# An attention, Fourier-mixing and gated feed-forward kernel: the last 64 tokens of two batches share one output tile, the gated part is unrolled, and the stages stand in a new order

## The reference, cut to what matters

```python
# attention: 4 batches x 8 heads, 576 tokens, head size 64
out_d = softmax(q_d @ k_d.T * scale) @ v_d        # on means over 4 tokens, repeated 4 times
out_l = softmax(q @ k.T * scale, |i - j| < 4) @ v # local band
x = transpose(out_up + out_l)                     # 4 x 576 x 512
# mixing layer
u = x + real(fft(fft(x, axis=1), axis=2))
un = (u - mean(u)) / sqrt(var(u) + 1e-6)
x = u + relu(un @ w_ch1) @ w_ch2                  # 512 -> 2048 -> 512
# gated layer
h = relu(x @ w_in)                                # 512 -> 1024
conv = sum_k conv_w[k] * shift(h, k - 1)          # over tokens, 3 taps, zeros at the ends
out = (h * sigmoid(conv)) @ w_out                 # 1024 -> 512
```

## Time and profile before

| | us |
|---|---|
| median of 3 runs | 891.83 |
| lowest, highest | 890.42, 895.41 |
| profiled execution | 889.25 |
| its span, first to last instruction | 887.4 |

### The profile page before, as it was taken

The page is one execution under the profiler, slowest core; times in us unless marked ns, Lnnn a source line. Parts: engine busy times, 40 slices in busy tenths (PEclk is TensorE's granted clock), DMA queues, the critical chain, the costliest instruction groups (busy, mean ns, idle before and its releaser), DMA issues.

```text
span 887.4 us, 17493 instructions
## 1 busy us (share of the span) xinstructions
PE 855.7 (96%) x6884; PEld 792.4 (89%) x6884; DVE 474.4 (53%) x889; ACT 333.6 (38%) x1040; POOL 266.8 (30%) x272
## 2 busy tenths in 40 slices
...
GB/s 181 271 90 61 69 88 65 38 52 110 70 25 69 40 51 69 119 1 25 24 154 91 30 31 30 30 31 31 31 31 1 1 54 2 2 51 0 53 0 54
DMA packets 75492, 49.41 MB, mean 56 GB/s; under 512 B 59201, under 2 KB 64601, under 8 KB 75418
## 3 DMA queue, kind: packets, MB, share of 16 engines
...
...
## 4 chain that ended last, share of the span: by engine, by line
PE 82%; DVE 7%; ACT 4%; issue 2%; POOL 1%; SPq 1%; DMA 1%; ACTq 0%; DVEq 0%; POOLq 0%
PE banks L744 21%; PE banks L761 21%; PE banks L860 13%; PE banks L845 10%; PE banks L702 3%; PE banks L675 3%; PE banks L592 2%; PE banks L651 2%; PE banks L717 1%; PE banks L573 1%; ACT prob L901 1%; PE banks L614 1%; DMA qk_in<-in_q 1%; ACT cent L963 1%; PE banks L635 1%
## 5 line engine op out<-in xcount | busy, mean ns | idle before, releaser
L1199 DVE SCALAR_TENSOR_TENSOR hL<-banks,hH 128x256 fp32r<-128x256 f32 x144 | 60.3, 419 | 185.6 <-ACT hH L959 185.6
L959 ACT ACTIVATE hH<-banks 128x256 fp32r<-128x256 f32 x144 | 55.1, 383 | 253.3 <-PE banks L744 253.1
L1486 POOL TENSOR_TENSOR astage<-astage,rstd_bc 128x1024 f32<-128x1024 f32 x9 | 21.6, 2399 | 228.8 <-DVE astage L1329 228.8
L744 PE MATMUL banks<-unH,w1aH 128*128 128x256 f32 x288 | 86.9, 302 | 2.2 <-DVE hL L1199 2.1
L761 PE MATMUL banks<-hH,w2aH 128*128 128x256 f32 x288 | 83.6, 290 | 0.0
L744 PE MATMUL banks<-unH,w1bH 128*128 128x256 f32 x288 | 82.5, 287 | 0.0
L744 PE MATMUL banks<-unL,w1bH 128*128 128x256 f32 x288 | 82.1, 285 | 0.0
L761 PE MATMUL banks<-hH,w2bH 128*128 128x256 f32 x288 | 82.0, 285 | 0.0
L761 PE MATMUL banks<-hL,w2bH 128*128 128x256 f32 x288 | 82.0, 285 | 0.0
L761 PE MATMUL banks<-hH,w2bL 128*128 128x256 f32 x288 | 82.0, 285 | 0.0
L744 PE MATMUL banks<-unH,w1bL 128*128 128x256 f32 x288 | 82.0, 285 | 0.0
...
## 6 DMA issues: line engine op xcount, KB each, us to landing
...
acc_dram<-astage SPq DMA_DIRECT2D x9, 512.0 KB, 2.6
astage<-acc_dram SPq DMA_DIRECT2D x9, 512.0 KB, 3.3
out<-ostage SPq DMA_DIRECT2D x4, 1024.0 KB, 4.4
w2araw<-in_moe_w_ch SPq DMA_DIRECT2D x4, 512.0 KB, 8.2
```

Of the source, the lines that this page charges most:

```text
L744: last = nc.tensor.matmul(bank[0][:, 0:CT], w[wp][:, t, P * m:P * m + P], (unH, unL)[xp][:, t, :], start=(t == 0 and i == 0), stop=(t == P ...
L959: nc.scalar.activation(hH[:, m % 2, :], bank[0][:, 0:CT], ACT.Relu).then_inc(hH_ok, 1)
L1199: nc.vector.scalar_tensor_tensor(hL[:, m % 2, :], bank[0][:, 0:CT], 0.0, hH[:, m % 2, :].bitcast(F32), ALU.max, ALU.subtract).then_inc(hL_ ...
L1486: nc.gpsimd.tensor_tensor(astage[:], astage[:], rstd_bc[:].unsqueeze(1).to_broadcast([P, PB, CT]), ALU.mult).then_inc(scaled, 1)
```

## The change

It has three parts.

The unpaired tile of 64 tokens goes. Rounded parts of a batch's last 64 tokens are kept for all 8 slices in `remH` and `remL`, an even batch's in the first 64 columns and the following odd batch's in the other 64. The odd batch contracts these 128 tokens as one tile, before its own four, and two stores take it out. Full tiles and the remainder are rounded by separate instructions.

The gated loop over batches is written out for every engine, and each tile gets its own store, which waits only for its own copy.

`PLAN` is replaced by another order of the same stages, with other counts of fillers (81 calls before, 69 after). Nothing else is added to it or taken from it. The diff of `PLAN` is some 150 lines; here its start stands, and then the places of which the prediction speaks, from the new list.

```diff
-        NTO = (S + P - 1) // P
-        SPAD = NTO * P
+        FULL = S // P
+        REM = S - FULL * P
+        SF = FULL * P
         NG = 4
-        hgH = sb("hgH", [P, NG, SPAD], F32R)
-        hgL = sb("hgL", [P, NG, SPAD], F32R)
-        ostage = sb("ostage", [P, NTO, D])
+        hgH = sb("hgH", [P, NG, SF], F32R)
+        hgL = sb("hgL", [P, NG, SF], F32R)
+        remH = sb("remH", [P, M2, 2 * REM], F32R)
+        remL = sb("remL", [P, M2, 2 * REM], F32R)
+        ostage = sb("ostage", [P, FULL + 1, D])
...
+        def o_tiles(b):
+            return (FULL, 0, 1, 2, 3) if b % 2 else (0, 1, 2, 3)
...
-            with sp.Fori(0, B) as b:
-                sp.wait_ge(o_kept_a, 3 * b + 3)
-                sp.wait_ge(o_kept_v, 2 * b + 2)
-                full = S // P
-                sp.dma_start(out[b][0:full * P].rearrange("(t p) d -> p t d", p=P),
-                             ostage[:, 0:full]).then_inc(o_stored, 16)
-                sp.dma_start(out[b][full * P:S], ostage[0:S - full * P, full]).then_inc(o_stored, 16)
+            for b in range(B):
+                for i, tt in enumerate(o_tiles(b)):
+                    if tt % 2:
+                        sp.wait_ge(o_kept_v, 2 * b + tt // 2 + 1)
+                    else:
+                        sp.wait_ge(o_kept_a, kept_a(b) + (1 if tt == FULL else tt // 2 + 1 + b % 2))
+                    if tt < FULL:
+                        sp.dma_start(out[b][P * tt:P * tt + P], ostage[:, tt]).then_inc(o_stored, 16)
+                    else:
+                        sp.dma_start(out[b - 1][SF:S], ostage[0:REM, tt]).then_inc(o_stored, 16)
+                        sp.dma_start(out[b][SF:S], ostage[REM:P, tt]).then_inc(o_stored, 16)
...
-                for tt in range(NTO):
+                for tt in o_tiles(b):
...
                     for i, (wp, xp) in enumerate(THREE):
-                        last = nc.tensor.matmul(bank[tt][:, :], (hgH, hgL)[xp][:, m % NG, P * tt:P * tt + P],
-                                                (woH, woL)[wp][:, m, :], start=(m == 0 and i == 0),
+                        tokens = ((hgH, hgL)[xp][:, m % NG, P * tt:P * tt + P] if tt < FULL else (remH, remL)[xp][:, m, :])
+                        last = nc.tensor.matmul(bank[tt], tokens, (woH, woL)[wp][:, m, :], start=(m == 0 and i == 0),
                                                 stop=(m == M2 - 1 and i == 2))
...
-                        nc.scalar.copy(hgH[:, n % NG, 0:S], hg[n % 2][:]).then_inc(hgH_ok, 1)
+                        nc.scalar.copy(hgH[:, n % NG, :], hg[n % 2][:, 0:SF])
+                        nc.scalar.copy(remH[:, n, REM * (b % 2):REM * (b % 2) + REM], hg[n % 2][:, SF:S]).then_inc(hgH_ok, 1)
...
-            for slots in (hgH, hgL):
-                nc.vector.memset(slots[:, :, S:SPAD].bitcast(F32), 0.0).then_inc(slots_zero, 1)
...
-                        nc.vector.tensor_tensor(hgL[:, n % NG, 0:S], hg[n % 2][:], hgH[:, n % NG, 0:S].bitcast(F32),
+                        nc.vector.tensor_tensor(hgL[:, n % NG, :], hg[n % 2][:, 0:SF], hgH[:, n % NG, :].bitcast(F32),
+                                                ALU.subtract)
+                        nc.vector.tensor_tensor(remL[:, n, rem], hg[n % 2][:, SF:S], remH[:, n, rem].bitcast(F32),
                                                 ALU.subtract).then_inc(hgL_ok, 1)
```

More of the change, by code:

```diff
@@ L84 @@
[L84 to L113, removed]
@@ L119 @@
[L119 to L133, removed]
@@ new lines @@
+    flip_k.3.0 keep_up.1 flip_k.3.1 keep_k.3.0 round_w1.0.1 weigh.1.0 pool_q.3 load_k.4 keep_k.3.1 pool_k.3 flip_p.2.0
+    pool_v.3 join.1.0 score.3.0 keep_p1.2.0 keep_p0.2.0 score.3.1 mask.3.0 low_w1.0.0 load_vg.4 top_l.3.0 flip_p.2.1
+    mask.3.1 weigh.1.1 exp_l.3.0.0 wmeans.0.1 top_l.3.1 load_vw.3 keep_p1.2.1 low_w1.0.1 top_d.3.0 exp_l.3.0.1
+    keep_p0.2.1 top_d.3.1 exp_d.3.0.0 exp_l.3.1.0 join.1.1 flip_pd.2 fold.1 centre_w1.0.2 exp_l.3.1.1 centre_w1.0.3
+    keep_pd.2 exp_d.3.0.1 flip_q.4.0 flip_q.4.1 exp_d.3.1.0 invert.3.0 pooled.2 load_q.5 exp_d.3.1.1 norm_l.3.0
@@ new lines @@
+    join.3.0 exp_l.4.0.1 flip_k.5.1 keep_k.5.0 load_k.6 weigh.3.1 top_d.4.1 round_w2.0.1 join.3.1 load_vw.5 fold.3
+    pool_q.5 exp_d.4.1.0 exp_d.4.1.1 round_w2.0.2 pool_v.4 fold_d.0.1 invert.4.0 low_w1.0.3 warm.15.1 feat.0.0.0
+    keep_k.5.1 load_vg.5 pool_k.5 feat.0.0.1 keep_cos.0.0 feat.0.1.0 top_l.4.1 keep_sin.0.0 norm_l.4.0 low_w2.0.1
+    exp_l.4.1.0 score.5.0 flip_p.4.0 exp_l.4.1.1 feat.0.1.1 keep_cos.0.1 mask.5.0 keep_p1.4.0 feat.0.2.0 keep_sin.0.1
+    invert.4.1 top_l.5.0 norm_l.4.1 feat.0.2.1 keep_cos.0.2 exp_l.5.0.0 keep_p0.4.0 turn.0.0 seq.0.0.0 top_d.5.0
@@ new lines @@
+    load_k.7 norm_d.5 keep_k.6.0 seq.0.3.1 keep_k.6.1 pool_k.6 mix_p.0.2 flip_p.5.0 keep_qs.0.3 join.4.0 score.6.0
+    keep_p1.5.0 mix.0.3 norm_l.5.1 weigh.4.1 keep_p0.5.0 mask.6.0 mix_p.0.3 load_vw.6 flip_p.5.1 join.4.1 keep_p1.5.1
+    keep_p0.5.1 top_l.6.0 flip_pd.5 fold.4 round_u.0.0 round_u.0.1 low_u.0.0 keep_pd.5 low_u.0.1 top_d.6.0 round_u.0.2
+    flip_q.7.0 round_u.0.3 flip_q.7.1 low_u.0.2 pooled.5 exp_d.6.0.0 low_u.0.3 load_q.8 exp_d.6.0.1 expand.0.0
+    keep_up.5 pool_v.7 exp_l.6.0.0 score.6.1 relu.0.0 exp_l.6.0.1 split.0.0 load_vg.8 weigh.5.0 top_d.6.1 keep_q.7.0
```

285 lines of the change are left out of this document (159 added, 126 removed).

## The result

| | before | after |
|---|---|---|
| median of 20 runs each, same chip (us) | 891.12 | 884.88 |
| lowest to highest | 889.03 to 901.21 | 878.67 to 890.00 |
| profiled execution, its span | 889.25, 887.4 | 886.86, 885.1 |
| mean granted clock in it | 0.982 | 0.967 |

The ratio is 0.9916 (95%: 0.9891 to 0.9941): 7.5 us less by it, 6.2 by the medians, where the prediction gave 18.2 and a range that ended at 881. The gain is in the gated part and at the end. The new order of stages, which was to give 4.9 us, costs some 7.

What follows compares the result with a forecast made beforehand. TensorE, holding 82% of the chain of waits, was taken to bound the kernel. Savings of 11.2 + 2.1 + 4.5 + 0.4 = 18.2 us from the runs' median of 891.83 gave 873.6 us, range 867 to 881.

Steps and rivals of the forecast that it cites:

- The shared tile: Gated part: 432 matmuls instead of 480, 48 fewer at a pitch of 0.2333 us, 11.2 us saved, lower bound 5.8.
- rival 4: Gated part: a matmul that goes frees only a narrow one's pitch, 0.120 us; 879.0 us in all, chance 0.03.
- The split: Gated part: separate instructions add 0.1 us per slice on VectorE or ScalarE, covered by waits; cost 0, at worst 8.
- unrolling: Gated part: writing out the loop wins nothing and costs 0, though more distinct instructions must be fetched.
- Rival 5: Gated part: unrolled code is fed too slowly; 14 ns more per pair cost 17 us, 20 ns give 898; chance 0.03.
- Stores and end: After TensorE's last matmul: a smaller last store lands sooner, 2.1 us saved, bounds 0 and 2.5.
- End of the layer norm: At the layer's end: one centring step stays before the square, which then waits for a relu; 0.4 us saved.
- The front: Before the first transform matmul: the new order closes holes of VectorE; 4.5 us saved, bounds -4 and 7.3.
- sign of being wrong: The first transform matmul starting at 79 us or later, where about 75 was forecast.
- The middle: From 107.8 to 450 us: only 5.6 us of rest can be won; gain 0, bounds -3 and 3.
- to be paid back: Front: three stages slipping behind the transform's start gain some 1.8 us there, an estimate, to be lost again behind it.
- Rival 2: Front or middle loses 4 to 9 us through delayed loads or a lowered clock: 882 to 887, chance 0.08.

Runs made afterwards that it cites:

- e8: The kernel before with the gated part's loops written out for all four batches, nothing else changed: 893.36 us, ratio 1.0010.
- e12: e1 with the stores of the kernel before: 882.3 us, ratio 0.9902.
- e1: The kernel after with the PLAN of the kernel before: 877.0 us, ratio 0.9833.
- e13: The kernel after with the order of before only from the first transform stage to the first expansion: 880.72 us, ratio 0.9875.
- e3: The kernel after with load_vg.2 issued ahead of load_q.3: 884.3 us, ratio 0.9897.

## Why the prediction was wrong

- **The shared tile: right.** 11.2 us forecast, 11.15 in the chain, 432 matmuls. The pitch is 0.233 us, so rival 4 is out. The Trainium skill's figure in "TensorE: Matmul & The Clock Gate", section Back-to-back issue gap, 131 ns, would have made it an estimated 6.3: the trace disagrees.
- **The split, unrolling: right at 0.** The 64-column subtraction took 0.22 us (0.2 assumed). TensorE doesn't rest from its first contraction to its end. Rival 5 is out by e8.
- **Stores and end: right.** 2.1 forecast; the span ends 4.1 us after the last matmul where it was 5.9, so 1.8 less, and 2.3 by the traces of e12 and e1.
- **End of the layer norm: as forecast.** The relu (L977) starts at 460.61 and the square at 460.89, 0.28 us apart; in the earlier trace rows it is 0.74.
- **The front: the step that failed.** "GpSimd's floor near 73 and VectorE's 79.5 - 5.5 = 74 put the transform at about 74 to 75.5; I take 4.5 us." It came at 87.05 here, behind the 79 that the prediction named as its sign of being wrong, and at 84.7 on average with a new front. The 79.56 it started from was itself the earliest of seven kernels with the old front, whose mean is 82.8. So the term was a loss of 1.8 us on average, not a gain of 4.5. Two holes of one timeline were summed and closed, as if the next instructions had had their operands. They hadn't: VectorE, TensorE and ScalarE release each other in turn here. From 28 to 88 us in the kernel after, ScalarE waits 9.2 us for VectorE's masks and maxima, TensorE 2.8 for ScalarE's `probdT`, and VectorE 17.4 for TensorE, where it was 11.1; all of VectorE's rests are 60 - 41.9 = 18.1 us against 60 - 46.2 = 13.8.
- **The middle: priced at nothing.** "Only 5.6 us of rest can be won, and TensorE's work is the same: 0, bounds -3 and 3" was said of 107.8 to 450 us and holds there. But 79.6 to 107.8 us, which lies in neither term, was priced only by the front's remark that its slipped work is "to be paid back". Its new order costs 4.9 us net by the traces, 3.7 by the times of e13. Nor did the prediction have a price for the lower clock that followed, 0.84 for 0.90 in this stretch.
- **Rival 2** comes nearest, with 882 to 887 and a chance of 0.08; of its mechanisms, the later load of v is not it by itself (e3), and the lower clock has a share whose size is open. By the traces the change is 11.2 + 2.3 - 6.7 = 6.8 us, with the end of the layer norm inside the 6.7, against 7.5 measured.
